# Attention and two FFNs on one core: the gate and value products of the second FFN as seven block products, their shared sums added by DVE

## The reference

```python
# 1. attention, 2 batches, 8 heads, 768 positions, head_dim 64: position i sees the
#    first 8 positions and those with 0 <= i - j < 96, with a bias by distance
scores = where(keep, q @ k.T / 8 - slope[h] * dist, -1e9)
x = softmax(scores) @ v                      # (1536, 512)
# 2. first FFN, d_ff 1024
h = x @ w_in
solu = h * softmax(h)
y = ((solu - mean) / sqrt(var + 1e-6) * g_ln) @ w_out
# 3. second FFN, d_ff 1536
yn = y / sqrt(mean(y * y) + 1e-6) * rms_g
out = (silu(yn @ w_gate) * (yn @ w_val)) @ w_down
```

## Time and profile before

| | us |
|---|---|
| median of 3 runs | 592.25 (591.99 to 592.34) |
| the profiled execution | 591.57 |
| its span, first to last instruction | 589.8 |

### The profile page before, as it was taken

One profiled execution on the slowest core, in us unless ns is written; L12 is line 12 of the kernel. 1 busy time (PEld: TensorE's weight loads), 2 busy tenths in 40 slices (PEclk: granted clock), 3 DMA queues, 4 the chain that ended last, 5 costly groups with the idle time before them and its releaser, 6 DMA issues.

```text
span 589.8 us, 10771 instructions
## 1 busy us (share of the span) xinstructions
PE 558.5 (95%) x3697; PEld 480.2 (81%) x3697; DVE 307.1 (52%) x790; ACT 265.5 (45%) x610; POOL 93.9 (16%) x223
## 2 busy tenths in 40 slices
PE   2786999999999999999999999999999999999997
PEld 1564777777777777768899999999999999999996
DVE  4769878877887898767465132222212222222221
ACT  3668666776677786746443212222221222222112
POOL 4541122124202223323000010000001000000000
PEclk9997999999999999999999999999999999999999
DMA  8656662444244422414340200020020000001000
GB/s 216 193 148 183 198 174 77 125 125 125 76 125 125 127 76 76 159 57 176 111 170 9 73 1 1 1 72 0 1 72 0 0 0 36 0 0 37 1 1 36
DMA packets 21613, 46.95 MB, mean 80 GB/s; under 512 B 2764, under 2 KB 2776, under 8 KB 21576
## 3 DMA queue, kind: packets, MB, share of 16 engines
q1 hardware_dynamic: 21264, 46.47, 26.2%
q10 hardware_dynamic: 312, 0.01, 0.0%
HBM read 40.18 MB, written 6.29 MB: 79 GB/s over the span
## 4 chain that ended last, share of the span: by engine, by line
PE 80%; DVE 10%; POOL 4%; issue 3%; ACT 1%; DMA 1%; ACTq 0%; DVEq 0%; SPq 0%
PE hidden L413 9%; PE hidden L414 8%; PE hidden L415 8%; PE mixed L1265 3%; PE turned L413 3%; PE turned L414 3%; PE mixed L413 3%; PE scores_a L413 3%; PE mixed L414 3%; PE scores_b L413 3%; PE scores_a L414 3%; PE scores_b L414 3%; PE scores_b L415 3%; PE scores_a L415 3%; PE turned L415 3%
## 5 line engine op out<-in xcount | busy, mean ns | idle before, releaser
L741 ACT ACTIVATE act_hi<-act_sb 128x256 fp32r<-128x256 f32 x72 | 30.2, 420 | 108.8 <-DVE act_sb L1121 108.8
L1121 DVE TENSOR_TENSOR act_sb<-mixed,silu 128x256 f32<-128x256 f32 x36 | 15.3, 425 | 94.1 <-PE mixed L415 93.9
L1121 DVE TENSOR_TENSOR act_sb<-turned,silu 128x256 f32<-128x256 f32 x36 | 15.3, 424 | 88.6 <-PE turned L415 85.9
L413 PE MATMUL hidden<-down_hi,act_hi 128*128 128x512 f32 x144 | 56.9, 395 | 0.1
L414 PE MATMUL hidden<-down_lo,act_hi 128*128 128x512 f32 x144 | 56.9, 395 | 0.0
L415 PE MATMUL hidden<-down_hi,act_lo 128*128 128x512 f32 x144 | 56.7, 394 | 0.0
L685 ACT ACTIVATE probs_t<-turned 116x512 f32<-116x512 f32 x48 | 28.7, 598 | 54.9 <-PE turned L1250 54.9
L1126 DVE TENSOR_TENSOR act_lo<-act_sb,act_hi 128x256 fp32r<-128x256 f32 x72 | 30.6, 426 | 35.0 <-ACT act_hi L741 35.0
L675 ACT ACTIVATE probs<-logits,neg_max 128x232 f32<-128x232 f32 x96 | 45.8, 481 | 6.0 <-DVE neg_max L1008 6.0
L413 PE MATMUL hidden<-in_hi,xt_hi 128*128 128x512 f32 x96 | 42.8, 446 | 0.9 <-DVE xt_lo L1031 0.5
L413 PE MATMUL turned<-yt_hi,val_hi 128*128 128x256 f32 x144 | 40.8, 283 | 0.0
(11 more groups left out here) (147 smaller groups left out, 1540.2 us busy)
## 6 DMA issues: line engine op xcount, KB each, us to landing
qk_raw<-qk_pairs SPq DMA_DIRECT2D x96, 180.0 KB, 3.2
v_in<-v_windows SPq DMA_DIRECT2D x12, 448.0 KB
staging<-w_gate SPq DMA_DIRECT2D x3, 1024.0 KB, 7.4
staging<-w_val SPq DMA_DIRECT2D x3, 1024.0 KB, 5.8
y_spill<-y_out SPq DMA_DIRECT2D x12, 256.0 KB, 3.9
staging<-w_down SPq DMA_DIRECT2D x3, 1024.0 KB, 5.9
y_in<-y_spill SPq DMA_DIRECT2D x6, 512.0 KB, 3.9
out<-o_sb SPq DMA_DIRECT2D x12, 256.0 KB, 2.1
```

Source lines behind the costliest of these rows:

```text
L413: pe.matmul(acc, hi, other_hi, start=first, stop=False)
L741: nc.scalar.activation(act_hi[:, slot], act_sb[:, slot], ACT.Copy).then_inc(act_rounded, 1)
L1121: nc.vector.tensor_tensor(act_sb[:, slot], val_ps[slot][:, 0:WIDE], silu[:, slot], ALU.mult).then_inc(act_ready, 1)
```

## The change

The second FFN's gate and value products are no longer plain sums over four blocks of 128 features. The step is now 512 tokens by 256 gate and 256 value columns (`FF = 256`, `TOKENS = 512`), seen as a 2 x 2 x 2 block product: features in two halves of 256, tokens in two halves of 256, and the columns as gate and value. It is made from seven block products instead of eight, in Winograd's form: P1 to P7, each of a factor of the weights and a factor of y that are halves, or sums and differences of halves. There are 6 groups of columns by 3 blocks of tokens, 18 steps.

- POOL makes the sums and differences: `sum_y(b)` four adds of 128x512 for each of the three token blocks, `sum_w(j)` four for each of the six column groups.
- ACT and DVE split seven factors of each (`round_y`/`split_y`, `round_w`/`split_w`). rms_g is now multiplied into y (`scale_y`, four ACT copies a tile) and not into the weights.
- Of the seven product banks ACT copies P1; DVE adds all the others from PSUM: `gate_1`, `sum_u2`, `sum_w`, `sum_u3`, `val_2`, `val_1`, `gate_2`. The sums u2 and w, which several outputs share, are among these.
- The output products of a group are added to `out_acc` in SBUF by DVE (`add_out`), since a column group now runs over all tokens before the next begins; all stores of the output stand at the end.
- Block 0 of y (tiles 0 to 3) is loaded, normalised, transposed, summed and split in tiles 6 to 10 of the attention stage; the weights of group 0 in tiles 10 and 11. The loop of `one_tile` ends two tiles earlier (`LOOP_TO = tiles - 6`). The order between the stages is written anew on every engine.

The diff, cut to its core (in `_(dve)`, `sum_w(s)` is the sum of products; in `_(pool)`, `sum_w(j)` the sums of weights):

```diff
-        LOOP_FROM, LOOP_TO = 2, tiles - 4
+        LOOP_FROM, LOOP_TO = 2, tiles - 6
...
+        turn_at = {(7, 0): 0, (7, 1): 1, (8, 0): 2, (8, 1): 3, (11, 3): 4}
+        round_y_at = {(8, 2): 0, (8, 3): 1, (9, 0): 2, (9, 1): 3, (9, 2): 4, (9, 3): 5, (10, 0): 6}
+        split_y_at = {divmod(pairs * t + p + 1, pairs): i for (t, p), i in round_y_at.items()}
+        round_w_at = {(11, 0): (0, 1, 2, 3), (11, 2): (4, 5, 6)}
+        split_w_at = {(11, 0): (0, 1, 2, 3), (11, 3): (4, 5, 6)}
+        NORMALISE_AT = {(6, 3): 0, (7, 3): 1, (10, 3): 2, (11, 2): 3}
+        SCALE_AT = {(6, 0): 0, (6, 3): 1, (7, 3): 2, (10, 3): 3, (11, 3): 4}
...
+            def sum_w(j):                                       # POOL
+                added = w_sums(j)
+                g1, g2, v1, v2 = w_raw[:, 0, 0:2], w_raw[:, 0, 2:4], w_raw[:, 1, 0:2], w_raw[:, 1, 2:4]
+                at = 4 * j
+                pool.wait_ge(w2_loaded, 32 * (j + 1))
...
+                pool.tensor_tensor(added[:, 0], g1, v1, ALU.subtract).then_inc(w2_summed, 1)
+                pool.wait_ge(w2_summed, at + ADD_1)
+                pool.tensor_tensor(v1, v1, v2, ALU.add).then_inc(w2_summed, 1)
...
             for t in range(tiles):
+                if t == tiles - 1:
+                    newton_y(4)
                 newton(t)
...
+                if t == 5:
                     newton_y(0)
+                    newton_y(1)
+                if t == 6:
+                    newton_y(2)
+                if t == 7:
+                    sum_y(0)
+                if t == 9:
+                    newton_y(3)
+                    sum_w(0)
+            sum_y(1)
+            newton_y(5)
+            sum_y(2)
+            sum_w(1)
+            with pool.Fori(2, groups) as j:
+                sum_w(j)
...
+            def one_step(j, b, more):                           # DVE
...
+                split_act(s - 1, 1)
+                if b == 0:
+                    split_w(j, P4)
+                    split_w(j, P3)
+                if b == 1:
+                    split_down(j)
+                gate_1(s)
+                for i in (P1, P2) if ahead else ():
+                    split_w(j + 1, i)
+                sum_u2(s)
+                if ahead:
+                    split_w(j + 1, P6)
+                sum_w(s)
+                if ahead:
+                    split_w(j + 1, P5)
+                sum_u3(s)
+                val_2(s)
+                add_out(*before, 0)
+                if ahead:
+                    split_w(j + 1, P7)
+                add_out(*before, 1)
+                val_1(s)
+                gate_value(s, 0)
+                gate_2(s)
+                split_act(s, 0)
+                add_out(*before, 2)
+                gate_value(s, 1)
+                add_out(*before, 3)
...
+            gate_1(0)                                           # DVE, behind the last tile
+            apply_norm(tiles - 1)
+            sum_u2(0)
+            normalise_y(4)
+            split_y(1, 0)
             split_ln(tiles - 1, 0)
...
+            def widen(j, b, i):                                 # TensorE
...
+                if i == P1 and not first:
+                    pe.wait_ge(corner_added, CORNERS * (s - 1) + VAL_2)
...
+                if i == P6 and not first:
+                    pe.wait_ge(corner_added, CORNERS * (s - 1) + GATE_2)
...
+                if i == P4:
+                    pe.wait_ge(corner_added, CORNERS * s + GATE_1)
+                if i == P3:
+                    pe.wait_ge(corner_added, CORNERS * s + SUM_U2)
+                for f in range(2):
+                    cols, here = slice(f * P, (f + 1) * P), slice(f * HALF_T, (f + 1) * HALF_T)
+                    for k in range(2):
+                        ins = product(pe, product_ps[i][:, here], w7_hi[:, i, k, cols], w7_lo[:, i, k, cols],
+                                      yt_hi[b][:, i, k], yt_lo[b][:, i, k], k == 0, k == 1)
+                ins.then_inc(product_ready, 1)
...
+            def one_step(j, b):                                 # TensorE
+                before = (j, b - 1) if b > 0 else (j - 1, blocks - 1)
+                for i in (P1, P2, P6, P5, P7):
+                    widen(j, b, i)
+                narrow(*before, 0)
+                narrow(*before, 1)
+                widen(j, b, P4)
+                widen(j, b, P3)
+                narrow(*before, 2)
+                narrow(*before, 3)
...
+            for i in (P2, P6, P5, P7):                          # TensorE, second block of group 0
+                widen(0, 1, i)
+            turn_y(10)
+            narrow(0, 0, 0)
+            turn_y(11)
```

More of the change, by code:

```diff
@@ new lines, in _ @@
+            val_2(0)
+            for place in range(2, 4):
+                split_y(1, place)
+            val_1(0)
+            gate_value(0, 0)
+            for place in range(4, PRODUCTS):
+                split_y(1, place)
+            split_down(0)
+            split_act(0, 0)
+            scale_of_y(5)
+            gate_2(0)
+            gate_value(0, 1)
+            split_act(0, 1)
+            gate_1(1)
+            split_y(2, 0)
+            sum_u2(1)
+            normalise_y(5)
+            split_y(2, 1)
@@ new lines, in _ @@
+            sum_w(1)
+            sum_u3(1)
+            val_2(1)
+            add_out(0, 0, 0)
+            add_out(0, 0, 1)
+            split_y(2, 2)
+            val_1(1)
+            gate_value(1, 0)
+            gate_2(1)
+            split_act(1, 0)
+            for place in range(3, 5):
+                split_y(2, place)
+            add_out(0, 0, 2)
+            gate_value(1, 1)
+            add_out(0, 0, 3)
+            for place in range(5, PRODUCTS):
+                split_y(2, place)
@@ L1225, in _ @@
+            one_step(0, 2, True)
+            for b in range(blocks):
+                one_step(1, b, True)
+            with dve.Fori(2, groups - 1) as j:
+                for b in range(blocks):
+                    one_step(j, b, True)
+            for b in range(blocks):
+                one_step(groups - 1, b, False)
+            split_act(steps - 1, 1)
+            for i in range(4):
+                add_out(groups - 1, blocks - 1, i)
         @block.tensor
@@ new lines, in narrow @@
+            def narrow(j, b, i):
+                s = blocks * j + b
+                half, cols = i // 2, slice(i % 2 * P, (i % 2 + 1) * P)
+                pe.wait_ge(act_split, 2 * s + half + 1)
+                if b == 0:
+                    pe.wait_ge(down_split, 2 * (j + 1))
+                if known(s) and s == 0 and i < 2:
+                    pe.wait_ge(ln_steps, LN_STEPS * (tiles - 1) + 2)
+                else:
+                    pe.wait_ge(out_added, 4 * s + i - 1)
+                for f in range(2):
+                    ins = product(pe, o_ps[i % 2], act_hi[:, half, f, cols], act_lo[:, half, f, cols],
+                                  down_hi[:, f], down_lo[:, f], f == 0, f == 1)
```

703 lines of the change are left out of this document (421 added, 282 removed).

## The result

The changed kernel takes 586.81 us (median of 4 runs, 585.97 to 587.23) against 592.12 us of the kernel before on the same chip: a ratio of 0.9909 (95% interval 0.9894 to 0.9924), faster by 5.3 us. The forecast was a gain of 11. The profiled execution took 585.97 us with a span of 584.2, against 591.57 and 589.8 before.

The account below looks back on a forecast made before the run. TensorE was taken to bound both the attention stage and the second FFN. 591.6 - 25.5 + 3.5 + 5.5 + 2 + 3.5 - 0.4 = 580.2, taken as 581 us; range 571 to 590, the forecast's own 574 to 588 (chance 0.60).

Parts of the forecast that it names:

- the stalls outside the steps: Sign of being wrong: stalls outside the second FFN's steps under 5 or over 20 us in all.
- the steady part: Second FFN's steps: 15.5 us each, DVE's 12.5 us hidden under TensorE, 216 fewer matmuls gaining 25.5 us.
- B: Rival, chance 0.09: DVE bounds the steady part, steps of 16.0 to 16.1 us against 15.5; 592 us.
- Tile 10's layer norm: Attention stage: newton(10) queued on POOL behind newton_y(3) and sum_w(0); 5.5 us added, idle 6.5, ends 0 and 11.
- A: Rival, chance 0.17: nearly all added work is hidden, only 3 us of stalls are left; 570 us.
- D: Rival, chance 0.03: products run no faster in halves of 256 columns, TensorE's pitch rises by an eighth; 592 us.
- C: Rival, chance 0.11: POOL's 128x512 adds cost 2.4 us, three chains through its sums grow by 4.8 each; 599 us.
- the term of the handover: From attention to the second FFN: late layer norm, y of tile 11 and splits add 3.5 us, ends 0 and 12.
- two turn_ln(11): Handover: both wait about 1.5 us more than the 0.70 before, behind added DVE work.
- P6 of the second block: Handover: it needs the sixth of seven splits, gated by POOL's sum_y; 0.2 to 1 us.
- turn_y(10): Handover: y of tile 11, stored, reloaded and normalised, comes 1.8 us after TensorE wants it.
- The attention stage: Tiles 6 to 11: y norm, scale copies and sums moved in add 3.5 us, between 0 and 7.

Follow-up runs that it names:

- e3: Changed kernel with POOL's newton(10) ahead of sum_w(0) and group 0's summed weight factors rounded and split later in tile 11; 583.76 us, ratio 0.9847.
- e1: Changed kernel with POOL's sums of y and w cut to 4 of 256 columns, plain halves as factors, output not the reference's; 573.33 us, ratio 0.9683.
- e7: Changed kernel with the layer norm's steps ahead of the y norm's on DVE and POOL in tiles 6, 7 and 10, sum_w(0) last; 585.27 us.
- e10: e5 with e7's order on tile 10 alone and DVE also doing the four sums of w's first group; 576.5 us, ratio 0.9749.
- e12: e5 plus twelve POOL products of two SBUF tensors (128x512) on memory nobody else reads; 590.52 us, ratio 0.9982.
- e2: e1 with four small dependent POOL operations ahead of each small sum, to last about as long as a full sum; 576.61 us, ratio 0.9751.
- e6: Changed kernel with each step's two shared sums done by POOL from ACT's copies, not by DVE from PSUM; 586.6 us, ratio 0.991.
- e5: Changed kernel with twelve late sums (y's second and third block, w's second group) moved from POOL to DVE; 581.41 us, ratio 0.9815.
- e4: Changed kernel with DVE's split_ln(11) ahead of normalise_y(4) and the y splits, and POOL's sum_w(1) after the third block's splits; 584.35 us, ratio 0.9865.
- e8: e5 and e7 together in one kernel; 581.74 us, ratio 0.9822.
- e9: e5 with ACT scaling y tile 8 ahead of the second block's last factor, scale_of_y(5) ahead of its split on DVE; 582.46 us, ratio 0.9835.

## Why the prediction was right, and where it failed

The time lies inside the range given, but the stalls outside the steps come to 20.4 us (4.2 + 5.8 + 2.4 + 8.0), where over 20 was named as a sign of being wrong. The direction, the steady part and the first two stalls were right in size. The steps are 15.5 us (15.45 to 15.56), DVE is at 39.2 of 50, inside the 38 to 42 given, and no wait of TensorE stands there; so B falls. The split row held for the sums from PSUM (0.68). Tile 10's layer norm idled 6.81 us where 6.5 was given, ended by apply_norm and with newton behind four adds. Of the 5.8 added there, sum_w(0) makes 3.6 (e3, e1) and the y norm's steps ahead another 0.9 (2.27 in e7 and e10). A is refuted as the changed kernel stands. Of the 20 us that the added work costs on TensorE's path, POOL's sums make two thirds: 13.4 go with them in e1, and 6.7 are left there (0.9683 x 592 less 566.5). D falls with the step.

C, "slower: POOL", had the right engine and a wrong price. An add took 1.28 us at the least and 1.83 at the most, not 2.4. It is in both directions that one stops the other, and DVE's side of it is what reached TensorE.

The step that failed is the term of the handover: "Value 3.5", measured 8.0. Of its three parts the two turn_ln(11), "about 1.5 us more", took 2.35 more (3.05 against 0.70). P6 of the second block, "0.2 to 1 us", and turn_y(10), 1.8, took nothing: no wait of TensorE stands between 296 and 329. In their place P6 of the third block took 3.47, which the sum put at nothing without giving a reason (only rival C names that block's sums), and the fall of the clock behind it took 1.5, not charged either. That two parts too high stood against two left out is luck; without it the term would have been some 6 us short and not 4.5. The turn_ln part and the missing one have one reason. I had the row that shows the hold, a k_lo split of 1.98 us in place of 0.636 beside POOL, and used it in two places: in the steady part, where it is harmless, and at tile 10. At the handover I counted POOL's sums only as something that others wait for. There DVE is the engine that is late, and e12 shows that the hold by itself costs 9 to 10 us for twelve instructions of POOL on top of e5, and e2 that without it both waits go.

The Trainium skill ("SBUF — State Buffer", section "SBUF: two separate sides") has the pair locked for a whole instruction against DVE operations with two SBUF inputs or in a two-port mode. On the first the traces agree (1.52 and 1.75 under POOL's adds against 0.68 wherever one operand is in PSUM). normalise_y and apply_norm read one SBUF tensor each and are held as well (2.33, 1.78); that they run in a two-port mode no run here shows. "DVE would lose at most POOL's 4.8 us" was a true bound on DVE's time; it says nothing about TensorE's.

The attention stage's +4.0 against 3.5 was right in size. That the order of DVE's steps caused it, as I had argued, is not supported: e7 turned that order round and the stage got no shorter. Of its four waits of 0.86 to 0.90, the trace has two (at 186 and 208) ended by the last of ACT's four scale copies (`scale_y`): turn_ln waits for `turned_x`, as the prediction had it, 1.8 us together. The other two (179 and 201) are ended by DVE's split of the next q and k; what makes that late, the added load on DVE or ACT's queue behind the copies, stays open.

## What to carry to other kernels

- When POOL gets two-tensor SBUF work, list the DVE instructions that will stand under it, mark those whose tensors are all in SBUF, and ask of each whether someone waits for it at once. In a stretch with slack the hold is free (e6); in a handover it cost more than the change's whole net gain (e12, e2).
- Giving the work to the busier engine can be the faster choice: DVE at 0.68 an add, with no hold, beat an idle POOL at 1.3 to 1.7 (e5).
- A reordering that removes one wait is worth what the next one leaves (e4, e8, e9); the remaining waits have to be read again after each edit.

## What the runs showed of the hardware

- The hold spares DVE operations with a PSUM operand: 0.68 to 0.69 us beside POOL's 1.29 (e6, e12), against up to 1.52 for the same shape with all tensors in SBUF. The row ahead of the forecast did not tell the two apart.
- It works against POOL too: its adds take 1.28 us at the least and 1.6 where DVE operations with all tensors in SBUF stand close together (318 to 323), and in the changed kernel the first, one-column operation of newton(10) takes 1.28 us beside a w split, where it takes 0.33 in e2 and in its repeats here:

```profile
265.95 1.28 POOL L654 TENSOR_SCALAR col<-seed_bits,col 128x1 f32<-128x1 f32 x1
...
268.00 0.33 POOL L654 TENSOR_SCALAR col<-col 128x1 f32<-128x1 f32 x1
```

- The clock is not a function of one wait's length. After 3.05 us of idle TensorE it stayed at 1.00 in the changed kernel (290 to 300) and was 0.82 to 0.84 in e3; after 2.27 it was 0.66 in e10 and 1.00 in e7; after 3.47 it went to 0.50, which is 1.2 of 2.4 GHz. A fall has to be looked for at each wait; in the changed kernel it cost 1.5 and 2.4 us where it came.
